# Five low parts of weights on POOL, a few steps in another order, and q and k rows summed inside TensorE's transposes

## What is computed

```python
q_d = q.reshape(B, H, Sd, factor, D).mean(axis=3)      # factor 4, Sd = 144; k_d and v_d alike
out_up = np.repeat(sm_attn(q_d, k_d, v_d), factor, axis=2)
mask = np.abs(pos[:, None] - pos[None, :]) < factor    # a band of 7
scores = np.where(mask, scale * np.matmul(q, k.transpose(0, 1, 3, 2)), -1000000000.0)
...
x = (out_up + softmax(scores) @ v), as (tokens, channels)
xn = x / rms * rms_g
x = (silu(xn @ w_gate) * (xn @ w_val)) @ w_out         # 512 -> 1536 -> 512
h = np.maximum(x @ w_in, 0.0)
return (s * (h * h) + b) @ w_out2                      # 512 -> 2048 -> 512
```

## Time and profile before

| | us |
|---|---|
| median of 3 runs (983.19 to 984.95) | 983.49 |
| the profiled execution, device time | 980.89 |
| its span | 978.9 |
| PE busy in it | 944.5 |
| DVE busy | 535.3 |
| POOL busy | 373.7 |
| ACT busy | 354.4 |

### The profile page before, as it was taken

One profiled execution on the slowest core, in us unless ns is written; L12 is line 12 of the kernel. 1 busy time (PEld: TensorE's weight loads), 2 busy tenths in 40 slices (PEclk: granted clock), 3 DMA queues, 4 the chain that ended last, 5 costly groups with the idle time before them and its releaser, 6 DMA issues.

```text
span 978.9 us, 13231 instructions
## 1 busy us (share of the span) xinstructions
PE 944.5 (96%) x5031; PEld 761.8 (78%) x5031; DVE 535.3 (55%) x813; ACT 354.4 (36%) x816; POOL 373.7 (38%) x192
## 2 busy tenths in 40 slices
PE   8788799989999999999999999999999999999998
PEld 4667699756777777777778998888888888888897
DVE  7888997876774765554532323434433443343343
ACT  3358855743225222422241434222222322222232
POOL 6767776767883876356600554000000000000000
PEclk9898899999999999999999999999999999999999
DMA  9986573523321331012013331102001100100010
GB/s 255 276 266 217 155 225 101 168 62 103 100 92 39 83 108 46 20 33 76 14 41 118 118 113 65 43 1 87 1 1 44 44 0 1 65 1 1 1 44 22
DMA packets 54380, 79.42 MB, mean 81 GB/s; under 512 B 9837, under 2 KB 37069, under 8 KB 52909
## 3 DMA queue, kind: packets, MB, share of 16 engines
q1 hardware_dynamic: 52284, 71.53, 24.2%
q10 hardware_dynamic: 2032, 7.05, 1.9%
HBM read 67.05 MB, written 11.50 MB: 80 GB/s over the span
## 4 chain that ended last, share of the span: by engine, by line
PE 81%; DVE 6%; DMA 4%; ACT 3%; issue 2%; SPq 1%; POOL 1%; ACTq 0%; DVEq 0%; POOLq 0%
PE bank L782 25%; PE bank L922 7%; PE bank L923 7%; PE bank L924 7%; PE bank L904 7%; PE bank L905 7%; PE bank L906 7%; PE bank L818 4%; PE bank L816 4%; PE bank L817 4%; ACT prod_a L578 1%; DMA vs<-in_v_dram 1%; DMA ks<-in_k_dram 1%; DVE x L606 1%; DVE sc L596 1%
## 5 line engine op out<-in xcount | busy, mean ns | idle before, releaser
L551 POOL TENSOR_TENSOR prod<-qs,ks 128x896 f32<-128x896 f32 x80 | 183.5, 2315 | 81.0 <-DVE sc L596 66.1
L565 POOL TENSOR_TENSOR prod<-sc,vs 128x896 f32<-128x896 f32 x72 | 136.7, 1998 | 64.4 <-DVE x L606 33.9
L945 DVE SCALAR_TENSOR_TENSOR r<-bank,r 128x512 f32<-128x512 f32 (+1 forms) x80 | 51.1, 638 | 181.0 <-ACT r L933 181.0
L906 PE MATMUL bank<-y_h,w2i_l 128*128 128x512 f32 (+1 forms) x320 | 117.8, 368 | 0.0
L933 ACT ACTIVATE r<-bank 128x512 f32<-128x512 f32 (+1 forms) x80 | 44.4, 555 | 181.9 <-PE bank L906 181.1
L838 DVE TENSOR_TENSOR bank<-bank,u 128x512 f32<-128x512 f32 (+1 forms) x66 | 39.6, 600 | 119.9 <-PE bank L782 114.3
L782 PE MATMUL bank<-x_h,wv_h 128*128 128x512 f32 (+1 forms) x264 | 99.8, 390 | 0.0
L596 DVE TENSOR_REDUCE sc<-prod 128x14 f32<-128x896 f32 x80 | 85.7, 1078 | 15.2 <-POOL prod L551 15.1
L816 PE MATMUL bank<-h_h,wo_h 128*128 128x512 f32 (+1 forms) x264 | 93.1, 353 | 0.0
L818 PE MATMUL bank<-h_h,wo_l 128*128 128x512 f32 (+1 forms) x264 | 92.7, 351 | 0.0
L817 PE MATMUL bank<-h_l,wo_h 128*128 128x512 f32 (+1 forms) x264 | 92.7, 351 | 0.0
(11 more groups left out here) (142 smaller groups left out, 1929.1 us busy)
## 6 DMA issues: line engine op xcount, KB each, us to landing
raww<-in_moe_w_out_dram SPq DMA_DIRECT2D x14, 512.0 KB, 4.1
ks<-in_k_dram SPq DMA_DIRECT2D x16, 280.0 KB
vs<-in_v_dram SPq DMA_DIRECT2D x16, 280.0 KB, 4.7
y_scr<-y_st ACTq DMA_DIRECT2D x4, 1024.0 KB, 5.4
raww<-in_moe_w_in_dram SPq DMA_DIRECT2D x8, 512.0 KB, 3.4
y_raw<-y_scr SPq DMA_DIRECT2D x4, 1024.0 KB, 4.8
out_dram<-o_st SPq DMA_DIRECT2D x16, 256.0 KB, 2.8
rawq<-in_q_dram SPq DMA_DIRECT2D x3, 1152.0 KB, 13.1
```

What stands on the lines that cost most here:

```text
L551: pool.tensor_tensor(dst, qv, kv, ALU.mult).then_inc(prod_ready, 1)
L565: pool.tensor_tensor(dst, pv, vv, ALU.mult).then_inc(prod_ready, 1)
L906: last = pe.matmul(o, w2i_l[:, m, kk, :], y_h[t % 2][:, kk, 0:w], start=False, stop=kk == DT - 1)
```

## The change

Four things are changed at once.

1. The low parts of pieces 2, 3, 7, 15 and 16 move from DVE to POOL. The low part of piece 1 stays on DVE but stands further back.
2. On ACT, `silu` of step 0 goes ahead of the high part of piece 4, and `hidden_hi` of step 15 ahead of the normalising of tile 1.
3. On DVE, `least(31)` goes ahead of the first qk sum of tile 1; `hidden_mul` of step 15 goes ahead of the inverse root; sums of tile 2 and the steps 16 and 17 are shuffled.
4. `pool_q` and `pool_k` of batches 1 to 3 are gone. PE waits for the load itself and turns all four quarters of a row, twelve transposes a unit instead of six, into the same PSUM tile.

```diff
@@ POOL
             weight_lo(pool, 0)
+            weight_lo(pool, 2)
             qk_mult(pool, 1, 2)
             qk_mult(pool, 1, 3)
+            weight_lo(pool, 3)
...
             qk_mult(pool, 1, 8)
+            weight_lo(pool, 7)
...
             weight_lo(pool, 14)
+            weight_lo(pool, 15)
+            weight_lo(pool, 16)
             weight_lo(pool, 17)
@@ ACT
+            silu(act, 0)
             weight_hi(act, 4)
-            silu(act, 0)
             weight_hi(act, 5)
...
+            hidden_hi(act, 15)
             normalise(act, range(FAC), 2)
-            hidden_hi(act, 15)
@@ DVE
-            pool_q(1)
...
-            pool_k(dve, 1)
...
             least(30)
-            weight_lo(dve, 1)
+            least(31)
             qk_reduce(dve, 1, 0)
             exponent_sums(3, 0)
             finish_pooled(2, 1)
-            least(31)
+            weight_lo(dve, 1)
...
-            weight_lo(dve, 3)
-            weight_lo(dve, 2)
             weight_lo(dve, 4)
...
-            weight_lo(dve, 7)
...
             add_pooled(dve, 1, 1)
-            weight_lo(dve, 15)
-            weight_lo(dve, 16)
+            hidden_mul(dve, 15)
             inverse_root_of(dve, 1)
-            hidden_mul(dve, 15)
@@ TensorE, turn_pooled
-                    pe.wait_ge(*((q_pooled, b) if kind == "q" else (k_pooled[b], 1)))
+                    pe.wait_ge((rawq_loaded if kind == "q" else rawk_loaded)[b], 16)
...
-                        for half in range(2):
-                            last = pe.matmul(to, raw[:, half * D:(half + 1) * D], ident[:, :], start=half == 0, stop=half == 1, is_transpose=True)
+                        for f in range(FAC):
+                            last = pe.matmul(to, raw[:, f * D:(f + 1) * D], ident[:, :], start=f == 0, stop=f == FAC - 1, is_transpose=True)
```

## The result

| | us |
|---|---|
| median of before beside it | 983.68 |
| median of the changed kernel | 980.71 |
| ratio, 95% interval | 0.9968, 0.9953 to 0.9983 |
| the profiled execution of the changed kernel, its span | 983.78, 982.0 |

The account below looks back on a forecast made before the run. PE was taken as the bound from 127.5 us on, so seam -5.3, start +3.6 and pooled stage -2.0 add to -3.7 us; from the median 983.49 that gives 979.8 us (chance 0.48), range 975.0 to 984.2.

Parts of the forecast that it names:

- The seam, -5.3: Before tile 1's first full-width gate: earlier root and low parts remove PE's stops, 5.3 us faster, bounds -6.1 and -2.5.
- The place where a page was set against the sum: Seam: POOL's parts could block DVE's add by up to 1.8 us; normalising would end at 208.1, still before 209.1.
- The start, +3.6: First matmuls: later low part 1 delays piece 4's load and gate 2, 3.6 us slower, bounds -1 and +4.5.
- The stop before gate 1: First matmuls: PE's 2.05 us stop closes; one of 4 to 6 us comes before gate 2, lower clock behind it.
- I add least 31 not before 110.6: DVE at the start: the assumed earliest time of least 31, from which low part 1 starts at 113.05 instead of 109.79.
- gate 0 later than 117.9: Start of the first matmuls: a stream beginning with gate 0 later than 117.9 us would show the prediction wrong.
- rival 2: Start: piece 4 is not late, the stop closes unreplaced, 1 us faster there; whole time 975.2 us; chance 0.17.
- The pooled stage, -2.0: First 117.9 us: DVE's adds replaced by PE transposes, 2.0 us faster, bounds -4.5 and +3.8.
- -2.8 us, and the v add with its store follows: Pooled stage, batch 1: least 8 at 35.4 instead of 38.22 us, with the v add following; -2.0 kept.
- The stop that should shrink: Pooled stage, PE's wait at the dv load of batch 2: from 3.67 to some 1.7 us, under 2.5 as sign.
- rival 1: Pooled stage gives nothing back, v's store and load set it: 0 to +1 us; whole time 984.1; chance 0.18.
- Rival 3: PE becomes the bound of the pooled stage: +3.8 us there, whole time 985.6 us; chance 0.10.

Follow-up runs that it names:

- e5: Changed kernel with least(31) and DVE's low part of piece 1 back in the order of before; 0.9967 (0.9947 to 0.9986) against before.
- e7: e5 with DVE's q and k adds and six transposes a unit as before; 0.9978 (0.9958 to 0.9997) against before.
- e9: e1 plus silu of step 0 ahead of the high part of piece 4; 0.9927 (0.9906 to 0.9948) against before, median 977.99 us.
- e1: Kernel before with the seam part alone (low parts 15, 16 on POOL; step 15's multiply and high part earlier); 0.9938 against before, 6.1 us faster.
- e4: Changed kernel without any edit, measured again on the chip of the single parts; 0.9975 (0.9952 to 0.9998) against before.
- e10: Repeat of e1, the seam part alone on before, on one chip with e9 and e11; 0.9959 (0.9943 to 0.9974), median 980.20 us.
- e11: Changed kernel again, on one chip with e9 and e10; 0.9962 (0.9945 to 0.9978) against before, median 980.33 us.
- e3: Kernel before with the start part alone: low parts 2, 3, 7 on POOL, low part 1 later, silu earlier; 1.0017 against before, 1.7 us slower.
- e2: Kernel before with the transposes alone: DVE's six q and k adds gone, twelve transposes a unit; 0.9999 (0.9975 to 1.0023) against before.
- e8: e2 with only six transposes a unit, so DVE's adds are gone and PE gets no added work; 0.9995 (0.9970 to 1.0021) against before.
- e6: Changed kernel with least(31) alone put back behind co, low part 1 staying late behind it; 0.9972 (0.9948 to 0.9995) against before.
- e12: e2 with every transpose of batches 1 to 3 made twice, 24 a unit; 1.0097 (1.0081 to 1.0113) against before, 9.6 us slower.

## Why the prediction came out right, and where it was not

The time of 979.8 was predicted and 980.7 measured; by sum -3.7 and -3.1 us. Only the first of the three steps is as good as that. (In the prediction's working two sums are 0.1 us off, 2.8 us to spare in the seam and 115.5 for the end of low part 1, and half of the spread of its bounds reaches up to 984.5, not 983.5. Nothing hangs on them.)

**The seam, -5.3: right.** Alone it gave -6.1 and -4.0 us, 5.1 in the mean, and C to D is shorter than before's by 5.6 to 6.1 us in six profiles that have it. In the other three (e5, e7, e9) it is shorter by 4.2 to 4.7, and there PE has a stop of 1.0 to 1.1 us behind C that before doesn't have. The root began 2.2 us behind the last add (2.3 was the sum's number), ACT waited 2.25 us for it ("2 to 3"), and all stops went but 0.3. The place where a page was set against the sum was the one that mattered: the prediction let the add keep its 1.23 us and noted that POOL's parts could block it by up to 1.8. In after, e1, e4, e9, e10 and e11 it takes 2.88 to 2.90 us, 1.65 to 1.67 more. That is the rule of the Trainium skill (SBUF — State Buffer, Who interferes with whom), and the trace agrees with it to the 1.0 us that remained between the normalising and PE (2.7 by the sum without the rule, 1.0 with it).

**The start, +3.6: the mechanism right, the place not, the size open.** The stop before gate 1 closed and one before gate 2 came, of 2.50, 2.15 and 3.91 us instead of 4 to 6, with some 3 us of the lower clock behind it as forecast. The failing step was "I add least 31 not before 110.6", 3.8 us behind the root: that was where PE's scores of head 31 ended in the one profile of before. In e11 it runs at the same distance (3.7 us behind the root), and low part 1 begins 6.05 us behind it, with 6.2 predicted. In after, e3 and e4 TensorE was at its lower level from 4.4 to 6.9 us ahead of A on, `least(31)` ran 5.5 us behind the root, and low part 1 began 7.9 behind. What the step had not followed at all is who else waits there: co stands behind `least(31)`, and behind co stand ACT's store of it, the exponents of head 31 and x_h. So gate 0 itself moved, by 2.6 us in after and e4 and by 1.8 in e3. By these profiles it takes both, the new order and the lower clock: in e1, e2, e8 and e9 the lower level also began 4.5 to 6.4 us ahead of A, and with the old order A to B stayed at 11.07 to 11.37; in e11 the order was new, the clock full until 1.1 us behind A, and it was 11.01. No run set the clock apart from the rest.

The prediction named one sign of being wrong that came: gate 0 later than 117.9. It came at 126.67, 121.74 and 121.40. But with the old start it came at 118.36 to 121.66 in e1, e2, e8 and e10, so this sign alone tells nothing of the change.

What gate 0 loses, gate 2 need not wait for. A to C is 27.45, 27.65, 26.11 and 28.46 us in the four profiles with the whole start part (after, e4, e11, e3), and 21.58 to 25.91 in the six with the old start: the two groups don't overlap, and the means are 3.8 us apart, near the 3.6 of the sum. The times give less and don't agree: +1.7 (e3), +3.6 (e4 against e1), +0.3 (e11 against e10). Only e1 and e10 had, with the old start, a stop before gate 1 as long as 3.4 to 3.7 us, and both are the seam alone; why is open. The silu move may have been priced too low as well, 1 us in rival 2 against 3.1 by the ratios of e9 and e10 (2.2 by the medians); but their intervals touch, and 1 us isn't excluded. Rival 2 is half true: with the order left alone piece 4 is issued 4.8 us ahead of gate 0 (118.98, e9), and it is e9 and not the changed kernel that comes nearest to its 975.2.

**The pooled stage, -2.0: not there.** The step that failed is "-2.8 us, and the v add with its store follows". least 8 ran at 35.77 to 36.22 us in e2, e5 and e6 and at 37.68 to 38.16 in after, e4 and e11 ("by 36" was the forecast), 1.3 us earlier in the mean than in the six profiles with DVE's adds. Where DVE was free early enough, the load of v of batch 1 had not landed (39.70 in after, 40.30 in e8); where it had (e2), the gain was gone by the next batch, and so it is in the mean of the six. The stop that should shrink did: at the values of batch 2 PE stands 0.6 us (ACT's) in after, e2, e5 and e11 and 2.5 and 2.4 in e4 and e6, against 2.3 to 4.0 with DVE's adds. That bought nothing. The stop at the values of batch 1, which looks in after as if it had grown from 1.47 to 4.53, can't be put down to the change: it is 0.4 to 4.5 us with DVE's adds and 0.6 to 4.5 with the twelve. All this fits rival 1, that v's load, store and load set the stage whenever the turns are made, but no run moved v's loads or its store, so it is argued and not shown. The rival had 0 to +1; measured -0.1 us (-2.5 to +2.3) for the part, -0.5 for e8, and -1.1 for e5 against e7.

So the seam was right, and of the 2.0 us of the stage most or all was missing. By the times of the single parts a start that cost 1.7 instead of 3.6 made up for it; by A to C it did not, and that the whole still came to -3.1 then leaves 1.7 us unexplained. Either way it is luck that the sum came out this near. Rival 3 is out at this size; with three times the added transposes (e12) PE has hardly any idle time left. What else stays open: why A varies over 5.6 us between executions of the same code, and why D to E is 753.4 us in all kernels with twelve transposes a unit or more and 753.7 to 754.4 in the others.

## What to carry to other kernels

Move work off an engine only where the engine was waited for: five low parts and six adds were moved here, and the two that stood between an add and a root brought all of the gain. The one move that may add to it was that of a step in front of a late transfer (silu ahead of a weight, e9). In a hand-written order ask of each step that is moved ahead not where it stands but when its operand is there; a wait put at the front delays everything behind it on that engine, and on the next. Where single executions differ by more than the effect, cut the profile at fixed points and compare the pieces, and take each piece from all the profiles that have it: one pair gave here a stop that grew by 3 us, and the other profiles don't bear it out.

## What the chip showed that I had not expected

- TensorE stayed at 1.2 GHz for 20.00 us while busy for 19.95 (after, 108.5 to 128.5), and from 101 to 124.5 us in e4 (busy for 19.15 of the 19.20 from 102.5 on). The work there is small matmuls (72 x 72, 144 columns and fewer) with fillers of 512 columns between. In after a stop of 2.20 us had ended 1.2 us ahead of it. In before and e11 the same kind of work ran at the lower level for only some 7 us (106.2 to 113 in before), in e1 and e9 for some 13.5. A busy PE in the row of the page doesn't tell its clock.
- Two low parts in a row on POOL stretch a two-input DVE instruction beside them from 1.21 to 3.16 us (e5 against e6; 3.15 in e7). One that starts just after such a part begins waits nearly all of it out: 2.88 for 1.23 us, and 2.86 to 2.90 in all nine profiles with the seam part.
